# Clustered attention with a token and channel mixer on one core: a new order of steps in the pair loop, denominators kept in the transposes' bank, and 16-bit idle work in the opening

## The reference

```python
q_assign = np.argmax(np.einsum('bhsd,hcd->bhsc', q_n, c_n), axis=-1)
k_assign = np.argmax(np.einsum('bhsd,hcd->bhsc', k_n, c_n), axis=-1)
mask = q_assign[:, :, :, None] == k_assign[:, :, None, :]
scores = scale * np.matmul(q, k.transpose(0, 1, 3, 2))
scores = np.where(mask, scores, -1000000000.0)
scores = scores - np.max(scores, axis=-1, keepdims=True)
attn = np.exp(scores)
attn = attn / (np.sum(attn, axis=-1, keepdims=True) + 1e-09)
out = np.matmul(attn, v)
...
x = mixer_1(out)    # relu(x^T W1) W2 over tokens, relu(u W1) W2 over channels
return mixer_2(x)   # theta = x W, cos and sin, two token products, relu(u W)
```

## Time and profile before

| | us |
|---|---|
| median of 3 runs | 657.24 |
| lowest and highest | 656.51, 659.72 |
| the profiled execution | 658.8 |
| its span (first to last instruction) | 656.7 |
| first scores start | 14.72 |
| last V of the attention starts | 245.13 |
| one pair in the loop | 28.2 |

### The profile page before, as it was taken

How to read it: one execution, slowest core, us unless ns; L and a number is a source line. 1 busy time by engine, 2 the same in 40 slices (tenths; PEclk the granted TensorE clock), 3 DMA queues, 4 the chain that set the end, 5 groups by cost and what they waited for, 6 DMA issues and landing times.

```text
span 656.7 us, 10677 instructions
## 1 busy us (share of the span) xinstructions
PE 649.1 (99%) x3932; PEld 576.1 (88%) x3932; DVE 342.2 (52%) x562; ACT 291.0 (44%) x527; POOL 157.9 (24%) x91
## 2 busy tenths in 40 slices
PE   8999999999999999999999999999999999999998
PEld 8767667776777768999999999999999999999997
DVE  6778787787878755343023023222488146561142
ACT  5777677776767754434012013013676045510010
POOL 5563314132257353044000000100324000060000
PEclk8999999999999999999999999999999999999999
DMA  6486555755356411022000000100431000000022
GB/s 219 99 211 175 148 108 137 173 109 156 84 143 131 145 50 49 1 56 106 0 1 1 1 0 0 48 0 3 143 97 64 1 1 0 1 1 1 0 97 97
DMA packets 18127, 46.91 MB, mean 71 GB/s; under 512 B 3152, under 2 KB 7248, under 8 KB 18096
## 3 DMA queue, kind: packets, MB, share of 16 engines
q1 hardware_dynamic: 18096, 46.48, 26.2%
HBM read 24.15 MB, written 3.15 MB: 42 GB/s over the span
## 4 chain that ended last, share of the span: by engine, by line
PE 91%; issue 4%; DVE 1%; POOL 1%; SPq 1%; DMA 1%; ACT 1%; POOLq 0%; ACTq 0%
PE ps L462 20%; PE ps L464 20%; PE ps L463 20%; PE ps L519 8%; PE ps L537 8%; PE ps L507 5%; PE ps L508 4%; PE ps L773 1%; PE ps L691 1%; PE ps L630 1%; PE ps L545 1%; DMA kb<-pair_s 1%; DVE neg_max L1184 1%; SPq L292 1%; PE ps L483 1%
## 5 line engine op out<-in xcount | busy, mean ns | idle before, releaser
L881 ACT ACTIVATE prob<-ps,neg_max 128x768 f32<-128x768 f32 x96 | 86.5, 901 | 38.8 <-DVE neg_max L1184 37.0
L1184 DVE TENSOR_REDUCE neg_max<-ps 128x1 f32<-128x768 f32 x96 | 90.6, 945 | 13.4 <-PE ps L508 12.6
L464 PE MATMUL ps<-u_s,ch_s 128*128 128x384 f32 (+1 forms) x256 | 85.5, 334 | 0.0
L462 PE MATMUL ps<-u_s,ch_s 128*128 128x384 f32 (+1 forms) x256 | 85.5, 334 | 0.0
L463 PE MATMUL ps<-u_s,ch_s 128*128 128x384 f32 (+1 forms) x256 | 85.5, 334 | 0.0
L1004 ACT ACTIVATE g_s<-ps 128x384 fp32r<-128x384 f32 x48 | 23.6, 492 | 139.4 <-PE ps L464 139.4
L519 PE MATMUL ps<-ident,prob 128*128 128x128 f32 x576 | 83.8, 275 | 0.7 <-ACT pt L846 0.5
L519 PEld LDWEIGHTS ps<-ident,prob 128*128 128x128 f32 x576 | 67.8, 141 | 16.5 <-issue 6.1
L507 PE MATMUL ps<-ka,qa 128*128 128x384 f32 x192 | 73.7, 384 | 0.4 <-ACT prob L881 0.3
L1320 DVE TENSOR_TENSOR act_u<-ps,act_u 128x384 f32<-128x384 f32 (+1 forms) x32 | 16.9, 555 | 99.7 <-PE ps L464 99.7
L538 PE MATMUL ps<-pt,v_s 128*64 128x384 f32 x192 | 68.8, 494 | 0.0
(11 more groups left out here) (162 smaller groups left out, 1305.5 us busy)
## 6 DMA issues: line engine op xcount, KB each, us to landing
stage<-ch_dram SPq DMA_DIRECT2D x9, 768.0 KB, 4.6
qa<-pair_s SPq DMA_DIRECT2D x30, 192.0 KB, 3.0
ka<-pair_s SPq DMA_DIRECT2D x30, 192.0 KB, 4.0
raw<-q_dram SPq DMA_DIRECT2D x8, 384.0 KB, 3.3
raw<-k_dram SPq DMA_DIRECT2D x8, 384.0 KB, 4.7
v_s<-v_dram SPq DMA_DIRECT2D x16, 192.0 KB, 2.4
out_dram<-act_u SPq DMA_DIRECT2D x16, 192.0 KB, 1.9
qb<-pair_s SPq DMA_DIRECT2D x15, 192.0 KB, 3.4
```

The source lines that it names most:

```text
L462: pe.matmul(o, a_lo, b_hi, start=start, stop=False)
L464: return pe.matmul(o, a_hi, b_hi, start=False, stop=stop)
L881: act.activation(prob[:, s % 2, :].rearrange("p (c k) -> p c k", c=2), ps[:, 2 * (s % 2):2 * (s % 2) + 2, 0:HS], ACT.Exp, bias=neg_max[:, ...
L1184: dve.tensor_reduce(neg_max[:, s % 12:s % 12 + 1], ps[:, slot:slot + 2, 0:HS], AX.XY, ALU.max, negate=True).then_inc(s_max, 1)
```

## The change

Four things are changed, all in the attention. (1) The first result of the denominators goes into unused columns of bank 5 (the bank of T1) instead of those of the score slot; the two small DVE instructions now stand in front of evict1(1) and evict1(9) instead of max(3) and max(11). (2) The order of steps on PE, ACT and DVE is new; three times in a pair two scores follow each other with nothing between them (6 and 7, 8 and 9, 10 and 11), `sims` stands alone between transposes, later than before, and V2 stands between T1(9) and T0(9). (3) In the last pair T0(9) comes ahead of V2. (4) `idle_work` uses bf16 transposes and more of them (8, 28, 10, 20, 14, 20 instead of 4, 16, 5, 12, 8, 10).

```diff
                 transposed(p, 1, 0, first_of_all=first)
                 if not first:
                     weighted_v(p - 1, 1, 1)
-                if not last:
-                    sims(p + 1)
                 transposed(p, 1, 1)
                 next_score(p, 3)
                 transposed(p, 0, 1)
+                transposed(p, 1, 2)
+                next_score(p, 4)
+                transposed(p, 0, 2)
+                if not last:
+                    sims(p + 1)
...
                 transposed(p, 1, 8)
+                transposed(p, 0, 8)
                 next_score(p, 10)
-                transposed(p, 0, 8)
+                next_score(p, 11)
                 transposed(p, 1, 9)
-                next_score(p, 11)
+                if last:
+                    transposed(p, 0, 9)
                 weighted_v(p, 1, 0)
-                transposed(p, 0, 9)
                 if not last:
+                    transposed(p, 0, 9)
                     next_score(p, 12)
                 transposed(p, 1, 10)
+                transposed(p, 0, 10)
...
             def idle_work(n, bank=1):
+                unread = ps[:, bank, 0:HS].bitcast(BF16)
                 for i in range(n):
-                    pe.transpose(ps[:, bank, (i % 4) * P:(i % 4 + 1) * P], ident[:], ident[:])
+                    pe.transpose(unread[:, (i % NT) * P:(i % NT + 1) * P], identb[:], identb[:])
...
                 evict(p, 8, first)
                 exp(p, 10)
-                if last:
-                    exp(p, 11)
+                exp(p, 11)
                 o_odd_out(n + 2)
                 evict(p, 9, first)
-                if not last:
-                    exp(p, 11)
                 evict(p, 10, first)
...
-            def row_max(p, s, half=None, of=0):
+            def row_max(p, s):
                 slot = 2 * (s % 2)
                 dve.wait_ge(s_score, 12 * p + s + 1)
-                if half is not None:
-                    denominators(of, half, ps[:, slot, HS:HS + NT])
...
-            def evict(p, s, first=False):
-                half, t = s // HT % 2, s % HT
+            def evict(p, s, first=False, half=None, of=0):
+                q_half, t = s // HT % 2, s % HT
                 dve.wait_ge(s_pt_pe[1], 12 * p + s + 1)
+                if half is not None:
+                    denominators(of, half, ps[:, 5, HS:HS + NT])
```

More of the change, by code:

```diff
@@ L579, in pair @@
                 transposed(p, 0, 1)
+                transposed(p, 1, 2)
[3 more added lines that the diff above has]
+                    sims(p + 1)
+                transposed(p, 1, 3)
+                next_score(p, 5)
+                transposed(p, 0, 3)
                 if not last:
                     sims_transpose(p + 1)
-                next_score(p, 4)
-                transposed(p, 1, 2)
-                transposed(p, 0, 2)
                 if not first:
                     o_transpose(p - 1, 1)
-                next_score(p, 5)
-                transposed(p, 0, 3)
-                transposed(p, 1, 3)
-                weighted_v(p, 0, 0, first_of_all=first)
[L591 to L597, removed]
+                transposed(p, 1, 4)
+                transposed(p, 0, 4)
+                next_score(p, 6)
+                next_score(p, 7)
+                transposed(p, 1, 5)
+                transposed(p, 0, 5)
+                weighted_v(p, 0, 0, first_of_all=first)
                 transposed(p, 0, 6)
                 transposed(p, 1, 6)
+                next_score(p, 8)
                 next_score(p, 9)
@@ L607, in pair @@
                 transposed(p, 1, 8)
+                transposed(p, 0, 8)
                 next_score(p, 10)
-                transposed(p, 0, 8)
+                next_score(p, 11)
                 transposed(p, 1, 9)
-                next_score(p, 11)
+                if last:
+                    transposed(p, 0, 9)
                 weighted_v(p, 1, 0)
-                transposed(p, 0, 9)
                 if not last:
+                    transposed(p, 0, 9)
                     next_score(p, 12)
                 transposed(p, 1, 10)
+                transposed(p, 0, 10)
                 if last:
                     token_in(0, 0)
-                transposed(p, 0, 10)
+                else:
+                    next_score(p, 13)
                 o_transpose(p, 0)
@@ L622, in pair @@
                     token_in(0, 1)
-                else:
-                    next_score(p, 13)
                 transposed(p, 0, 11)
@@ L638, in _ @@
             pe.wait_ge(s_oh_zero, 1)
-            idle_work(16)
+            idle_work(28)
             pe.wait_ge(s_cen_t, 2)
@@ L645, in _ @@
             for side in range(2):
-                idle_work(12 if side else 5)
+                idle_work(20 if side else 10)
                 pe.wait_ge(s_onehot, side + 1)
                 oh_transpose(bank=6 - side)
-            idle_work(8)
+            idle_work(14)
             next_score(0, 0, first_of_all=True)
             next_score(0, 1, first_of_all=True)
-            idle_work(10, bank=7)
+            idle_work(20, bank=7)
             def token_in(b, t):
@@ L924, in pair @@
                 evict(p, 2, first)
+                if not last:
+                    act.wait_ge(s_sim_pe, p + 1)
+                    copy(sim_rows[:], ps[:, 7, 0:HS]).then_inc(s_sim_rows, 1)
                 exp(p, 4)
@@ L927, in pair @@
                 exp(p, 5)
+                evict(p, 4, first)
+                evict(p, 5, first)
+                exp(p, 6)
+                exp(p, 7)
                 o_odd_out(n)
[L929 to L932, removed]
                 evict(p, 6, first)
+                evict(p, 7, first)
                 exp(p, 8)
-                evict(p, 7, first)
                 exp(p, 9)
+                o_odd_out(n + 1)
                 if not last:
                     rows_of_next(p, first)
-                o_odd_out(n + 1)
                 evict(p, 8, first)
                 exp(p, 10)
-                if last:
-                    exp(p, 11)
+                exp(p, 11)
                 o_odd_out(n + 2)
                 evict(p, 9, first)
-                if not last:
-                    exp(p, 11)
                 evict(p, 10, first)
@@ L1224, in pair @@
                 evict(p, 0, first)
-                if not first:
+                if first:
+                    evict(p, 1, first)
+                else:
                     row_max(p, 2)
[L1227 to L1231, removed]
+                    evict(p, 1, half=1, of=p - 1)
+                row_max(p, 3)
+                evict(p, 2, first)
+                row_max(p, 4)
                 if not first:
                     head_sum(p - 1, 1, 1)
+                evict(p, 3, first)
+                row_max(p, 5)
+                if not first:
+                    x_out(p - 1, 1)
+                evict(p, 4, first)
                 if not last:
                     argmax(p + 1, 0)
[L1236 to L1240, removed]
                     argmax(p + 1, 1)
-                row_max(p, 5)
+                row_max(p, 6)
+                row_max(p, 7)
+                evict(p, 5, first)
                 if not last:
                     argmax(p + 1, 2)
[L1245 to L1250, removed]
+                    argmax(p + 1, 3)
                 evict(p, 6, first)
                 head_sum(p, 0, 0)
-                if not last:
-                    argmax(p + 1, 3)
+                row_max(p, 8)
                 row_max(p, 9)
@@ L1259, in pair @@
                 evict(p, 7, first)
+                head_sum(p, 0, 1)
                 evict(p, 8, first)
-                head_sum(p, 0, 1)
                 row_max(p, 10)
-                row_max(p, 11, half=0, of=p)
-                evict(p, 9, first)
+                row_max(p, 11)
+                evict(p, 9, first, half=0, of=p)
                 head_sum(p, 1, 0)
@@ L1268, in pair @@
                 evict(p, 10, first)
+                if not last:
+                    row_max(p, 13)
                 evict(p, 11, first)
                 x_out(p, 0)
-                if not last:
-                    row_max(p, 13)
             for side in range(2):
```

6 lines of the change are left out of this document (2 added, 4 removed).

## The result

The changed kernel takes 665.1 us (median of 4 runs, 664.8 to 665.5) against 657.3 for the kernel before in the same comparison: a ratio of 1.0113, 95% interval 1.0093 to 1.0134. It is slower, as forecast, but 3.3 us slower than the forecast of 661.8 and above its range of 658.3 to 664.2.

A forecast was written before the change was run, and what follows sets the result against it. PE, busy 99% of the span, was taken to set the time. Terms of 6 x 0.75 + 1.6 - 1.15 - 0.2 = +4.75 us on the 657.24 median gave 662.0, forecast as 661.8, range 658.3 to 664.2.

The forecast's parts named there:

- the hole: Pairs 0 to 6, ahead of T0(10): PE waits 1.23 us for evict0(9), queued on ACT behind exp(11), which waits for T0(9).
- the -1.15 of pair 2: Pair 2: the wait of `sims` for POOL's copy of `cen_p` goes, saving 1.15 us, if it is in every run.
- The waits that go: Loop pair: PE's waits ahead of S(8) (0.28), V1 (0.11) and S(5) (0.14) all vanish, together -0.53 us.
- a lean of 0.08 to the good: Loop pair: 29.08 us taken as 29.0, since the change of kinds of PE work was thought to lean to the good.
- is worth nothing else: Denominators' new place on DVE: no gain of its own beyond exp(3)'s wait, already counted; exp(11) now waits for PE.
- Double scores and kinds of work: PE in a loop pair: doubles win 0.03 us, `sims` alone and V2 behind transposes cost; sum 0, ends -0.2 and +0.2.
- What follows the hole: Loop pair: later evict0(10) and exp(12) delay S(2), and denominators ahead of evict1(1) delay T1(2); +0.15 us, between 0 and 0.4.
- Pair 0: First pair: T1(1)'s wait stays bare and `sims` comes later at its own price; 1.6 to 1.8 us longer, taken as 1.6.
- Opening: Before the first scores: the new idle work ends sooner, -0.2 us; ends -0.9 and +1.5 if the clock comes up later.
- Last pair: Its `sims` never existed and waits change by some tenths in both directions: 0.
- taken from the middle: Whole sum: leaning values of two terms were taken from the middle, so 662.0 on the median became a forecast of 661.8.
- The rule of the Trainium skill that I weighed: Rival, chance 0.02: the clock falls in the hole, +3 us in each of seven pairs, 683 us.

The follow-up runs named there:

- the second experiment: The changed kernel with T0(9) ahead of V2 on PE in every pair, ACT's order staying as changed: 657.6 us, 1.0007 to the kernel before.

## Why the prediction was wrong in size and right in kind

The mechanism was right and the size was off. Two terms of the sum failed most: the hole, put at 1.23 and measured at 1.40, seven times 0.17 or 1.2 us; and the -1.15 of pair 2, a wait that was in the first profiled execution and not in the second, which took the median time.

*The hole.* Right in place, cause and chain; 1.40 instead of 1.23 us. Of the difference 0.13 are signals: I took 0.04 from PE to ACT and 0.05 from ACT to PE, the trace shows 0.08 and 0.14. The rest is 0.01 on ACT's chain and 0.03 because PE would have been at T0(10) a little sooner. The cause is shown by three kernels: one with the hole put in alone (+1.38 a pair), and two with it taken out in different ways.

*The waits that go.* I had 0.53 from three places, and a lean of 0.08 to the good: 0.61. A pair without waits takes 27.57 after the change, so against 28.22 before 0.65 were won. The sum was right, partly by luck, since the rows held more waiting than I read in them. I took 0.31 from oT to a score as the bare price; it is 0.25, so S(5) waited 0.20 and not 0.14, S(13) 0.06, and the six transposes ahead of oT 0.05. The waits were 0.70 in all. That the denominators' place "is worth nothing else" was wrong as well: by itself it wins 0.24 a pair.

*Double scores and kinds of work.* Put at 0, with a lean to the good. Measured, it is 0.04 the other way: 27.57 without waits after, and 27.98 - 0.28 - 0.11 - 0.06 = 27.53 in the kernel with only the denominators moved (its waits at S(8), V1 and S(13)). That is close to nothing.

*What follows the hole.* 0.15 expected, 0.21 measured (0.17 at T1(2), 0.04 at S(2)). The size was near, the reason mostly another: the 0.17 is the price of the denominators' new place and stays when the hole goes; only the 0.04 can follow the hole. With the hole's 0.17 this makes +0.96 a pair for +0.75: 1.3 us of the error over six pairs.

*Pair 2.* The step that had the least ground: "this wait goes: -1.15, if it is in every run". It was in one of the two profiled executions of the kernel before. The other five loop pairs, which all took 28.2, and a median 1.5 us below the profiled time spoke against it; I wrote the doubt down and still counted the credit in full against the median, where at most the share of runs that have it may be counted. 1.15 us of the error. Without it the forecast would have been about 663, 2 us low, and the range, moved up by 1.15 with it (an estimate), would just have held the 665.1.

*Pair 0.* +1.6 expected, +1.80 measured, at the end of my own bounds of 1.6 to 1.8 (0.2).

*Opening.* -0.2 expected, +0.16 measured (0.36). Idle work did end earlier, but the second ohT and what stands behind it met the low clock: it was low for no longer than before, but later (10.50 to 13.91, where the kernel before has 9.31 to 12.73). The end I gave for this was +1.5; three other profiles with this idle work start 0.8 to 1.9 us later than this one.

*Last pair.* 0 expected, +0.25 measured, of which 0.19 are a longer wait at T0(10) (0.72 against 0.53 by the bracket). And I took 0.2 off the sum for terms "taken from the middle", which had no ground.

Together 1.3 + 1.15 + 0.2 + 0.36 + 0.25 + 0.2 = 3.5, against 3.3 in the medians. All of these misses have the same sign; only the waits that go, 0.04 a pair better than counted, went the other way, and they are netted in the 1.3. Each term leaned to the smaller loss, so the range, built from the same terms, was too narrow above. The rule of the Trainium skill that I weighed (TensorE: Matmul & The Clock Gate, section A second HAM failure mode: psum-queue depth-cycling), that frequent short idle stretches between groups of matmuls can make the clock swing, did not show here: with a hole of 1.4 us in each of seven pairs the granted clock stayed at 1.00.

## What to carry to other kernels

When an instruction is moved ahead on an engine that works in order, read what it waits for and then everything that is queued behind it. Moving exp(11) ahead cost 1.4 us a pair, because it waited for T0(9) and the copy that PE needed stood behind it, on an engine that was 43% busy. Such a chain is priced well from the rows of the kernel before, if the signals are taken from measured gaps and not from guesses. A wait that is seen in one iteration of a loop and not in its neighbours may not be counted as a saving. And a step that is taken as a price without waiting should be read in several places: the 0.31 of oT was not one.

## What the runs showed of the hardware that I had not expected

- In the changed kernel 0.08 us pass from the end of the record of PE's transposes (128.96) to the start of the exp (129.04), and 0.14 from the end of ACT's copy (131.06) to PE's next transposes (131.20).
- Idle time behind a buffer's readers is put down to "issue" here (1.67 us ahead of exp(11)), although ACT waited for PE: exp(11) starts 0.08 behind the end of T0(9).
- In the opening of the changed kernel PE ran 32-column products (`L471`, 6.46 to 9.45) and then nothing but transposes. The granted clock fell from 2.4 to 1.2 GHz at about 10.50 and rose again at about 13.91, behind a stretch of transposes alone. The two times are worked out from the clock of the stretches of 1 us in which they lie:

```profile
10.00:11.00 1.00, 0.86 (x13) 0.75 1.05 436
...
13.00:14.00 1.00, 1.00 (x13) 0.54 0.00 0
```

- The granted clock doesn't tell all. In the profile of the second experiment it is 1.00 over the whole opening, and yet the 24 products took 5.33 us instead of 3.15, and the first score came at 16.56. Over the twelve profiles the first score started between 13.87 and 16.64; the 2.8 us between them are 0.4% of the time.
